# Retention, dense and routed FFN on one core: the first chunk's order and banks, the place of r's decay table, and the steps of the first two expert rounds

## What is computed

```
# 1: linear attention, B=4, H=8, S=768, D=48, per head
for t in range(S):
    y[t] = r[t] @ (state + (u * k[t]) outer v[t])
    state = w[:, None] * state + k[t] outer v[t]
# 2: dense FFN on the 3072 tokens (d_model 384, d_ff 2048)
h = x @ w_in
x2 = (max(h, 0) + alpha * min(h, 0)) @ w_out
# 3: 8 experts of 384 tokens each (d_ff 1024)
logits = x2 @ w_gate
# tokens go to experts greedily, by falling logit, each expert full at 384
out[token] = max(x2[token] @ w1[e], 0) @ w2[e]
```

## Time and profile before

| | |
|---|---|
| median of three runs | 841.37 us (841.29 to 842.76) |
| the profiled execution | 840.67 us, of which the span 838.8 us |
| TensorE matmul busy | 784.1 us, 93% of the span |
| VectorE busy | 515.3 us |
| GpSimd busy | 479.1 us |
| ScalarE busy | 209.0 us |
| mean granted TensorE clock | 0.972 of full speed |

### The profile page before, as it was taken

One profiled execution on the slowest core, in us unless ns is written; L12 is line 12 of the kernel. 1 busy time (PEld: TensorE's weight loads), 2 busy tenths in 40 slices (PEclk: granted clock), 3 DMA queues, 4 the chain that ended last, 5 costly groups with the idle time before them and its releaser, 6 DMA issues.

```text
span 838.8 us, 15944 instructions
## 1 busy us (share of the span) xinstructions
PE 784.1 (93%) x6314; PEld 655.0 (78%) x6322; DVE 515.3 (61%) x1040; ACT 209.0 (25%) x431; POOL 479.1 (57%) x469
## 2 busy tenths in 40 slices
PE   5789999999999999999999999938889999999996
PEld 3568777888788878887888888715779989989996
DVE  8886566666666566666665334476767777776221
ACT  1222311111111121112111211104144353353451
POOL 6688985555455545554554343208374775675871
PEclk9889999999999999999999999958999999999999
DMA  7584411222222222222000000014505515417401
GB/s 219 148 224 129 141 58 57 67 66 66 68 66 68 67 67 67 66 67 67 29 11 11 10 20 9 10 44 174 179 13 197 174 35 208 144 65 261 154 18 39
DMA packets 46648, 75.17 MB, mean 90 GB/s; under 512 B 6256, under 2 KB 31984, under 8 KB 46576
## 3 DMA queue, kind: packets, MB, share of 16 engines
q1 hardware_dynamic: 38176, 56.66, 21.3%
q10 hardware_dynamic: 5328, 8.06, 3.4%
q0 software_dynamic: 3072, 9.44, 3.1%
HBM read 64.71 MB, written 9.44 MB: 88 GB/s over the span
## 4 chain that ended last, share of the span: by engine, by line
PE 73%; DVE 9%; POOL 9%; issue 4%; DMA 2%; ACT 2%; SPq 0%; POOLq 0%; ACTq 0%; DVEq 0%
PE bank L1131 21%; PE bank L1133 19%; PE bank L1132 19%; POOL gl L448 3%; PE bank L1176 2%; PE bank L1147 2%; PE bank L1231 2%; PE bank L1159 2%; DVE grid L1029 2%; PE bank L1297 2%; POOL wout_l L388 1%; PE bank L1354 1%; DMA raw<-w 1%; DVE grid L1027 1%; POOL win_l L388 1%
## 5 line engine op out<-in xcount | busy, mean ns | idle before, releaser
L448 POOL TENSOR_TENSOR gl<-g,gh 128x512 fp32r<-128x512 f32 x96 | 127.5, 1329 | 210.5 <-ACT gh L573 210.5
L880 DVE TENSOR_SCALAR q<-bank,alpha_sb 128x512 f32<-128x512 f32 x96 | 72.1, 751 | 137.3 <-PE bank L1133 137.2
L573 ACT CAST gh<-g 128x512 fp32r<-128x512 f32 x96 | 59.6, 621 | 364.4 <-PE bank L1133 318.7
L1131 PE MATMUL bank<-gh,wout_h 128*128 128x512 f32 x288 | 120.2, 417 | 3.4 <-POOL gl L448 2.9
L1131 PE MATMUL bank<-xTh,win_h 128*128 128x512 f32 x288 | 113.9, 396 | 1.2 <-DVE xTl L771 1.2
L1133 PE MATMUL bank<-xTh,win_l 128*128 128x512 f32 x288 | 112.9, 392 | 0.0
L1132 PE MATMUL bank<-xTl,win_h 128*128 128x512 f32 x288 | 112.9, 392 | 0.0
L1133 PE MATMUL bank<-gh,wout_l 128*128 128x512 f32 x288 | 112.8, 392 | 0.0
L1132 PE MATMUL bank<-gl,wout_h 128*128 128x512 f32 x288 | 112.7, 391 | 0.0
L511 POOL TENSOR_TENSOR w1l<-raw,w1h 128x384 fp32r<-128x384 f32 x64 | 65.2, 1018 | 30.5 <-ACT w2h L628 30.4
L1131 PE MATMUL bank<-xeh,w1h 128*128 128x384 f32 x192 | 69.7, 363 | 0.4 <-DVE xel L961 0.4
(11 more groups left out here) (173 smaller groups left out, 1499.3 us busy)
## 6 DMA issues: line engine op xcount, KB each, us to landing
raw<-w SPq DMA_DIRECT2D x32, 768.0 KB
kt<-kT SPq DMA_DIRECT2D x48, 96.0 KB, 2.6
rt<-rT SPq DMA_DIRECT2D x48, 96.0 KB, 2.7
vs<-v SPq DMA_DIRECT2D x48, 96.0 KB, 2.9
vn<-v SPq DMA_DIRECT2D x24, 192.0 KB, 2.9
x2rows<-x2n SPq DMA_DIRECT2D x24, 192.0 KB, 1.9
kn<-kN SPq DMA_DIRECT2D x20, 192.0 KB, 2.4
rn<-rN SPq DMA_DIRECT2D x20, 192.0 KB, 2.6
```

The source lines that it names most:

```text
L448: nc.gpsimd.tensor_tensor(gl[:, f % 2], g[:, f % 2], gh[:, f % 2].bitcast(F32), ALU.subtract).then_inc(gl_ready, 1)
L573: nc.scalar.copy(gh[:, f % 2], g[:, f % 2]).then_inc(gh_ready, 1)
L880: nc.vector.tensor_scalar(q[:, f % 2], h, 0.0, alpha_sb[:, f:f + 1], ALU.min, ALU.mult).then_inc(q_ready, 1)
L1131: nc.tensor.matmul(o, a_h, b_h, start=first, stop=False)
```

## The change

Nothing of what is computed changes; there is one added instruction (a copy) and TensorE's number of idle matmuls ahead of chunk 0's FFN stays at 27. What moves:

- **r's decay table.** ScalarE copies `rpow` into bank 7, and `scale_r(0, 1)` and `scale_r(0, 2)` read the table there; `scale_r(0, 0)` and `scale_r(0, 3)` still read it in SBUF.
- **Banks of chunk 0.** Batch 2's new state goes to banks 3 and 4, batch 3's scores to banks 5 and 6, and turns 0 to 2 to bank 7. So `new_state(0, 2)` and `new_state(0, 3)` no longer wait for the masks of their batch.
- **Order of chunk 0** on all engines but SyncE, most of it below.
- **The last state update of chunk 0** goes from ahead of the FFN to behind `mask(1, 0)`, and `scores(1, 0)` waits for a mask in place of that update.
- **Bodies 0 and 1 of stage 3**: other steps for counts, digits, offsets, inverses and turns, and on VectorE `rows_lo(0, a)`, `relu_lo(0, 0)` and `relu_lo(0, 3)` each stand some instructions later.

```diff
         def score_bank(c, b, j):
-            return banks[1 + j] if first(c) and b % 2 else banks[5 + j]
+            return banks[1 + j] if first(c) and b == 1 else banks[5 + j]
 
         def state_bank(c, b, j):
-            return banks[3 + j] if first(c) and b == 0 else banks[1 + j] if first(c) and b % 2 else banks[5 + j]
+            return banks[(1 if b % 2 else 3) + j] if first(c) else banks[5 + j]
...
-            return banks[7 if not first(c) or b % 2 == 0 else 4][:, 0:DM].rearrange("p (k t) -> p k t", k=KD)
+            return banks[7 if not first(c) or b < 3 else 4][:, 0:DM].rearrange("p (k t) -> p k t", k=KD)
...
             own_products(0, 2)
             padded_keys(0, 2)
+            pool.wait_ge(rows_loaded[3], 32)
+            padded_keys(0, 3)
             own_products(0, 3)
             lo_piece(0)
+            lo_piece(1)
             own(0, 2)
-            padded_keys(0, 3)
-            lo_piece(1)
+            lo_piece(2)
             own(0, 3)
-            lo_piece(2)
             lo_piece(3)
...
             nc.scalar.copy(knpow[:], banks[7][:, 0:DM]).then_inc(knpow_ready, 1)
+            act.wait_ge(knpow_ready, 1)
+            nc.scalar.copy(banks[7][:, 0:TB], rpow[:].rearrange("p h t -> p (h t)")).then_inc(rpow_placed, 1)
...
-                    nc.vector.tensor_tensor(weights(c, b)[rows, j], rt[rows, b % 2], rpow[rows], ALU.mult).then_inc(rk_scaled, 1)
+                    decays = rpow[rows]
+                    if first(c) and b in (1, 2):
+                        dve.wait_ge(rpow_placed, 1)
+                        decays = banks[7][rows].rearrange("p (h t) -> p h t", h=H)
+                    nc.vector.tensor_tensor(weights(c, b)[rows, j], rt[rows, b % 2], decays, ALU.mult).then_inc(rk_scaled, 1)
...
-                if attention and i == 0:
-                    own(1, 0)
...
                             mask(i + 1, b)
+                            if i == 0 and b == 0:
+                                update(0, B - 1, 0)
+                                update(0, B - 1, 1)
+                                own(1, 0)
...
             scale(1, 0)
-            update(0, B - 1, 0)
-            update(0, B - 1, 1)
             dve.wait_ge(consts_loaded, 32)
...
-                if p == 1 and m == 2:
+                if p == 1 and m == 3:
                     for a in range(NA):
                         rows_lo(0, a)
+                if p == 1 and m == 4:
+                    relu_lo(0, 0)
...
-                    wait(pe, masked, 2 * b - 2)
-                    if b == 3:
-                        pe.wait_ge(s_updated, 4)
+                    if b >= 2:
+                        pe.wait_ge(masked, 2 if b == 2 else 6)
+                elif isinstance(c, int) and c == 1 and b == 0:
+                    pe.wait_ge(masked, 8)
...
-                pe.wait_ge(masked, 8 * c + 2 * b + 2)
+                if first(c) and b >= 2:
+                    pe.wait_ge(s_updated, 2 * b - 2)
+                else:
+                    pe.wait_ge(masked, 8 * c + 2 * b + 2)
...
-                counts_at = (2, 8, 19, 24, 29, 33) if new == 0 else (4, 8, 12, 16, 21, 25) if new == 1 else (2, 7, 11, 16, 21, 25)
+                counts_at = (2, 5, 10, 20, 25, 30) if new == 0 else (3, 7, 12, 17, 21, 25) if new == 1 else (2, 7, 11, 16, 21, 25)
-                inverses_at = (45, 47) if new == 0 else (38, 40) if new < E - 2 else (25, 27)
+                inverses_at = (42, 44) if new == 0 else (38, 40) if new < E - 2 else (25, 27)
```

More of the change, by code:

```diff
@@ L165, in build @@
         tables, tables_step, down_ready, idle_set = sem("tables"), sem("tables_step"), sem("down_ready"), sem("idle_set")
-        knpow_done, knpow_ready = sem("knpow_done"), sem("knpow_ready")
+        knpow_done, knpow_ready, rpow_placed = sem("knpow_done"), sem("knpow_ready"), sem("rpow_placed")
         stage_loaded = [sem(f"stage_loaded{n}") for n in range(3)]
@@ L599, in _ @@
             hi_piece(0, load=False)
+            first_half_state(2)
             hi_piece(1, load=False)
             turned_hi(0, 0)
-            first_half_state(2)
+            hi_piece(2, load=False)
+            first_half_state(3)
             turned_hi(0, 1)
-            hi_piece(2, load=False)
             load_piece(3)
+            turned_hi(0, 2)
             load_piece(4)
-            first_half_state(3)
-            turned_hi(0, 2)
+            turned_hi(0, 3)
             hi_piece(3, load=False)
             hi_piece(4, load=False)
-            turned_hi(0, 3)
             load_piece(5)
@@ L921, in _ @@
             update(0, 0, 1)
-            scale(0, 2)
+            scale_k(0, 2)
             update(0, 1, 0)
+            scale_r(0, 2)
             attended(0, 1)
@@ L928, in _ @@
             own(0, 2)
+            own(0, 3)
             update(0, 2, 0)
             attended(0, 2)
+            turned_lo(0, 0)
             mask(0, 3)
-            own(0, 3)
             update(0, 2, 1)
-            turned_lo(0, 0)
             turned_lo(0, 1)
@@ L1014, in while_placing @@
                     rows_lo(p - 1, 1)
-                if p == 1 and m == 3:
-                    relu_lo(0, 0)
             def search(p, level, k):
@@ L1050, in close @@
                 hold(V.tensor_tensor(logits[:], logits[:], over_tokens(closing, E), ALU.add))
-                if p >= 1:
-                    relu_lo(p - 1, 3 if p == 1 else 2)
+                if p >= 2:
+                    relu_lo(p - 1, 2)
             def slots(p):
@@ L1082, in route @@
                 inversion(p)
+                if p == 1:
+                    relu_lo(0, 3)
                 inversion_b(p)
@@ L1186, in turn @@
                     pe.wait_ge(x_ready, b + 1)
-                    pe.wait_ge(knpow_ready, 1)
-                    wait(pe, xl_ready, b - 1)
-                    if b == 1:
-                        pe.wait_ge(s_updated, 2)
+                    pe.wait_ge(rk_scaled, 9)
+                    if b == 3:
+                        pe.wait_ge(s_updated, 6)
+                    else:
+                        wait(pe, xl_ready, b)
                 else:
@@ L1262, in _ @@
             scores(0, 0)
-            busy(3, banks[0])
+            busy(1, banks[0])
             scores(0, 1)
             new_state(0, 0)
-            busy(2, banks[0])
+            busy(1, banks[0])
             attend(0, 0)
-            busy(1, banks[7])
+            busy(1, banks[5])
             new_state(0, 1)
-            pe.wait_ge(knpow_ready, 1)
-            busy(1, banks[7])
+            busy(1, banks[5])
             attend(0, 1)
-            busy(2, banks[7])
+            new_state(0, 2)
+            busy(2, banks[5])
             scores(0, 2)
             turn(0, 0)
-            busy(3, banks[3])
-            new_state(0, 2)
-            busy(1, banks[3])
+            pe.wait_ge(s_updated, 4)
+            busy(3, banks[1])
             attend(0, 2)
-            pe.wait_ge(s_updated, 4)
+            new_state(0, 3)
             scores(0, 3)
+            pe.wait_ge(x_ready, 3)
             turn(0, 1)
-            new_state(0, 3)
+            busy(3, banks[0])
             attend(0, 3)
             turn(0, 2)
-            busy(2, banks[3])
+            busy(1, banks[5])
             turn(0, B - 1)
-            busy(2, banks[3])
+            busy(4, banks[5])
             chunk(0, output=False)
```

8 lines of the change are left out of this document (4 added, 4 removed).

## The result

| | before | changed |
|---|---|---|
| median | 841.33 us (6 runs, 840.33 to 842.76) | 838.12 us (6 runs, 836.98 to 840.72) |
| profiled execution | 840.67 us | 840.72 us |

The ratio is 0.9963, 95% interval 0.9945 to 0.998: 3.2 us faster, half of the 6.4 us forecast. The profiled execution of the changed kernel is the longest of its six and as long as that of before, so its trace holds some 2.6 us that the median run doesn't have. The trace of before is one of seven of its first chunk's order that the experiments left, and the earliest of them at the first FFN matmul and at back(0, 2), so the others are named beside it there.

The account below looks back on a forecast made before the run. TensorE's matmuls were busy 93% of the span, so only its waits or low clock could pay. 840.67 - 3.0 (start) - 3.5 (stage 3) = 834.2 us profiled, median forecast 835.0, range 830.5 to 839.5.

Parts of the forecast that it names:

- The table in PSUM: Chunk 0's scale_r for batches 1 and 2: two multiplies take 1.40 us beside GpSimd, not 2.77 and 2.78.
- ScalarE's added copy is hidden: Chunk 0: the copy of rpow ends about when scale_r(0, 1) begins, at 13.64, so it costs nothing.
- mask(0, 3) near 33.5: Chunk 0 on VectorE: this mask comes 1.4 us earlier than 34.89, with scale_r(0, 3) losing 1.4 beside GpSimd.
- The first FFN matmul at 38.4: End of chunk 0's attention: the FFN begins 3.7 us earlier than 42.11, by 1.4 plus 2.3.
- The second shortening: From mask(0, 3) to the first FFN matmul: 2.3 us off the 7.2 us of before.
- 12.6 us from there to back(0, 0): First FFN matmul to back(0, 0): 12.6 us for 16.15, 3.5 more gained, a TensorE lead of 7.2.
- What of it passes on: Start of the kernel: how much of TensorE's 7.2 us lead survives, set by piece 8 coming 3.0 us earlier.
- first term -3.0: The start's share of the forecast: 3.0 us faster, taken from piece 8's lead, with bounds 1.0 and 5.0.
- its slower rival: Weight staging becomes a chain of loads, piece 8 lands at 61, TensorE waits: 845 us, chance 0.08.
- The wait at back(0, 2) that the prediction named: Chunk 0's FFN: TensorE, 7.2 us ahead, waits for GpSimd's gl there, maybe then at half clock.
- Stage 3, -3.5: Bodies 0 and 1: earlier search cuts body(1)'s waits from 4.8 to 1.3 us, 3.5 gained; bounds 1.0 and 4.8.
- one half pays: Rival: only stage 3 gains, 837.9 us, or only the start, 838.4; chance 0.15.

Follow-up runs that it names:

- psum_only: The kernel before with only r's decay table in PSUM for batches 1 and 2: 838.96 us, ratio 0.9975.
- after_again: The changed kernel measured once more, nothing altered, beside its variants: 838.73 us, ratio 0.9962.
- update_moved: The kernel before with only update(0, 3) and own(1, 0) moved behind mask(1, 0): 842.33 us, ratio 1.0009.
- loads_early: The changed kernel with the loads of pieces 3 and 4 issued right behind hi_piece(2): 835.94 us, ratio 0.9927.
- pool_order: The changed kernel with pieces 3 and 4 loaded early, chunk 1's loads spread and GpSimd's order changed: 831.93 us, ratio 0.9877.
- c0_only: The changed kernel without the stage 3 edits, so the first chunk's part alone: 841.92 us, ratio 0.9995.
- update_back: The changed kernel with update(0, 3) and own(1, 0) put back ahead of the FFN: 837.73 us, ratio 0.9953.
- s3_only: The kernel before with all edits of stage 3 alone: 836.83 us, ratio 0.9935.
- loads_spread: The changed kernel with pieces 3 and 4 loaded early and chunk 1's loads of batches 2 and 3 behind those batches' heads: 836.10 us, ratio 0.9938.

## Why the prediction was half right

**The table in PSUM: right.** The four multiplies took 0.70 each beside GpSimd, and mask(0, 0) came 1.2 us earlier (predicted 1.1); psum_only ends 2.4 us faster. The Trainium skill ("SBUF — State Buffer", section "Who interferes with whom") says that a VectorE instruction with at most one SBUF input and outside its two-port modes doesn't contend with GpSimd; the rows agree, 1.40 for 2.78. The dearer PSUM source that the prediction cites doesn't show: 1.40 with the table there or in SBUF. One step was put at nothing too soon: "ScalarE's added copy is hidden". In five of the ten traces with the changed start scale_r(0, 1) waits 0.90 us for it and starts 0.8 later, as in after_again; there the first FFN matmul starts between 41.40 and 41.67:

```profile
14.60 1.40 DVE L731 TENSOR_TENSOR g<-rt,bank 64x512 f32<-64x512 f32 x2 [0.90 <-ACT bank L595]
```

**mask(0, 3) near 33.5: wrong,** 34.44. scale_r(0, 3) did not meet GpSimd (1.41); scale_k(0, 3) did (1.80 for 0.69), and so did the first half of update(0, 2) (0.99 for 0.54), which together cost about what was forecast for scale_r. The sum for this mask left out that own(0, 3) and a turned_lo, 0.5 us each, now stand ahead of this mask. VectorE's waits are not the reason: from 13.6 to the mask they are 1.46 + 0.19 now, 1.17 + 0.51 before.

**The first FFN matmul at 38.4: a gain of 3.7, too large.** It was 40.84. In the kernels with the first chunk of before it started between 42.11 and 43.97 (median 43.5 of seven traces), in ten with the changed one between 40.84 and 41.96 (median 41.4): 2.1 us gained, and the trace that I read was the earliest of the seven. The second shortening, 2.3 us behind mask(0, 3), came to 0.8: attend(0, 3) took 1.86 at low clock and `attended` waited for it.

**12.6 us from there to back(0, 0): right only where the pieces come.** 12.5 in update_moved, 11.9 in loads_early, 12.3 in pool_order, but 15.6 in the changed kernel.

**"What of it passes on", first term -3.0: the step that failed.** It took piece 8 as the gate and 3.0 us as its lead. Piece 8's lead was 0.3, and the gate stood earlier: pieces 5 and 6, 3 to 4 us later than before, because the changed order asks for piece 4 in the full stretch. The prediction named that chain as its slower rival, but followed it only to piece 8 and TensorE. It holds GpSimd, whose queue has decay(1, 0) and gl(0) right behind those two low parts. The wait at back(0, 2) that the prediction named did come (2.00), but for this reason, and it left nothing of the lead. GpSimd has 14 us of work from there to gl(2); before, 3.1 us of gaps lay within it, now none, so whatever delay of decay(1, 0) goes beyond those gaps arrives at gl(2) whole. The term measured 0 (c0_only: 0.9995). The parts, each as measured apart: -2.4 for the table, and +2.2 for the loads of pieces 3 and 4, if what loads_early gives back is what they cost. The update gave +0.8 in the kernel before, with no change inside its interval, and nothing in the changed kernel (update_back), so the parts can't be added up closely.

**Stage 3, -3.5: right in its mechanism, a little small.** From chunk 1's first output tile to the stream's first matmul it is 436.5 us for 435.95 (after_again), 0.6 later for 0.5 predicted; body(1)'s waits are 1.2 for 1.3 predicted; behind the stream's start the traces give -4.4. What the prediction missed lies in body(0), which was to end "where it did, within 0.5". Reckoned back from body(1)'s first count by its wait and 0.52 us a step (an estimate from these rows), the stream takes 21.1 us there for 22.4, so that body(0) ends about 0.8 earlier: the many small waits that were forecast didn't come, one of 0.59 did (585.94). s3_only measured -5.0, interval -7.2 to -3.9 (841.84 times 0.9915 and 0.9954, less 841.84), so the 3.5 lies just outside it.

**The sum.** With 0 for the first term, 841.4 - 3.5 = 837.9 was in the text as the rival "one half pays", and 838.1 came. That it fits to 0.2 us is in part luck: with stage 3 at its measured -5.0 and the start at 0 it would be 836.4, and s3_only is at 836.8.

Open: how the changed start's own gain divides between the table, the banks and the rest of the order in pool_order. Only the table and the update were tried alone. Open as well: whether pool_order needs the spread loads, and how much of the start in the changed kernel is the wait for ScalarE's copy.

## What to carry to other kernels

When a change makes the critical engine earlier, follow the engine that feeds it through its whole in-order queue: add up its work, and the gaps in it, from the next instruction that the change can delay to the next one that is waited for. A DMA issue moved a few instructions, from an idle stretch of the DMA engines into a full one, can cost as much as the compute edit gains, above all where a staging buffer chains the following loads to it. An edit that measures nothing alone (the update) can be worth 2.4 us once the next gate is open, so try it again then.

## What was not expected of the hardware

- **Small differences in the clock at the start stay.** The same instructions put the first FFN matmul anywhere from 42.11 to 43.97. The first attend, for instance, took 1.14 us in the trace of before and 1.66 in s3_only's; VectorE then waited 1.14 for it. So one trace of such a stretch is good to about 1 us.
- **A wait costs TensorE twice.** Behind waits of 1.8 to 2.0 us at back(0, 2) the granted clock was 0.57 to 0.66 of full over the 4 us from there, and back(0, 3) came 6.7 us after back(0, 2), not 5.2: 1.5 us more (six traces, the changed kernel's and loads_spread's among them). In after_again, behind 1.32 us, and in update_back, behind 0.71, it was 5.2 at full clock.
- **A piece of 192 KB can take 6.3 us.** Piece 5, issued at 44.14 together with piece 6 beside chunk 1's loads (DMA share 1.10 and 1.06), was cast at 50.42 (7.2 us in after_again, 44.35 to 51.59). In loads_spread piece 6, issued at 42.55, was cast at 45.76, 3.2 us.
